# Attention of a fused kernel: scores in blocks of two steps on TensorE, unscaled q prepared on GpSimd

## The chip, the cores and the metric

The kernel runs on one core of one Trainium2 chip. The metric is the device time of one execution in microseconds (us); smaller is better. A core has TensorE (PE in the profile; its weight loads are PEld), VectorE (DVE), ScalarE (ACT), GpSimd (POOL) and SyncE (SP, which here only issues transfers). Each engine runs its own instructions in order, and waits on semaphores for the others.

## The reference

Three stages follow each other: a bucketed attention, a mixture of experts, and a token and channel mixing. Only the attention is touched:

```python
q_bits = (np.einsum('bhsd,dk->bhsk', q, proj) > 0)     # 6 sign bits for each row of q, and of k
mask = q_bucket[:, :, :, None] == k_bucket[:, :, None, :]
scores = scale * np.matmul(q, k.transpose(0, 1, 3, 2)) # scale = 1/8
scores = np.where(mask, scores, -1000000000.0)
scores = scores - np.max(scores, axis=-1, keepdims=True)
attn = np.exp(scores)
attn = attn / (np.sum(attn, axis=-1, keepdims=True) + 1e-09)
return np.matmul(attn, v)
```

There are 2 x 8 = 16 heads, 768 rows each, 64 columns.

## The kernel before

The 16 heads are worked on in 8 pairs. A head has 6 tiles of 128 query rows, so there are 96 steps g. Step g belongs to pair g // 12, to head g % 2 of it and to tile g % 12 // 2; n stands for g % 12. A step goes through four engines:

- PE, `score(g)`: four matmuls write `scores[g % 2]`, 128 query rows by 768 keys. Two multiply `q_aug` by `k_aug` (the high part of 64 columns, and 12 rows of sign bits that push a score far down where the buckets differ), two multiply `q_hl` by `k_lh` (the products of the low parts). It waits for the exponential of step g-2, which read the same buffer.
- DVE, `maximum(g)`: the negated row maximum `neg_max`, then `match` (is there a key in the row's bucket) and `bias`, each one column.
- ACT, `exponential(g)`: exp of `scores` times `match` plus `bias` to `probs[g % 3]`, with the row sums as a by-product.
- PE, `turn(g)`: six transposes of `probs` into `turned`, of which there is one buffer. It waits for the exponential of g and for the copy of g-1 out of `turned`.
- ACT, `evict(g)`: copies `turned` to `probs_t`.
- PE, `products`: 8 matmuls with v into `pv` in every odd step, for steps 8 and 9 back. Every six steps DVE copies `pv` to `out_t` (`evict_out`, at n = 2 and 8), PE turns that into `side` (`turn_out`, at n = 3 and 9), and DVE normalises it into `x_all`.

The order on ACT is written out: in iteration g first `evict(g - 2)`, then `exponential(g)`. The change leaves it as it is. The order on PE is `score(g)`, `turn(g - 2)`, and at odd g the products.

The next pair is prepared while the present one runs. GpSimd starts when the last scores of the pair before are done (`s_sc`), and makes `q_hl` (q times 1/8, rounded), the copies of k (`k_aug`, and half of `k_lh`) and `k_low`, for both heads. DVE makes `q_aug` and `q_low` (the low part of q) between its maxima. PE projects q and k on the bit directions at n = 5 (`Q_AT`) and n = 7 (`K_AT`) into `side`, and DVE turns them into bits (`signs`) at n = 5 and 6 for q, and at n = 7 and 8 for k; each call has two instructions (L268). Before PE writes `side` again, at n = 7 and in `turn_out`, `side_free` waits until the signs counted so far are read out of it:

```python
        def side_free(g):
            turns = (Q_AT < g % 12) + (K_AT < g % 12)
            pe.wait_ge(s_bits, min(8 * (1 + g // 12) + 4 * turns, 8 * NPAIRS))
```

The first pair is prepared apart, most of it on DVE, before the first step.

## Time and profile before

| | before |
|---|---|
| median of 3 runs | 756.32 us (755.98 to 756.4) |
| the profiled execution | 756.28 us, of which span 754.5 us |
| PE busy | 649.6 us (86%) |
| DVE busy | 441.1 us (58%) |
| ACT busy | 350.2 us (46%) |
| POOL busy | 290.3 us (38%) |
| first and last score matmul | 17.7 and 259.3 us |

The attention is the stretch up to about 273 us. Busy shares are of the whole span. A busy PE isn't PE at its peak, since matmuls are pipelined and their ends are modelled; the starts in the timeline are the better guide.

### The profile page before, as it was taken

To read this page: it belongs to the slowest core of one execution; us is meant where nothing else is said; L and a number is where in the kernel's file an instruction comes from. 1 tells how busy PE (TensorE), PEld (TensorE's weight loads), DVE (VectorE), ACT (ScalarE), POOL (GpSimd) and SP (SyncE) were. 2 spreads that over 40 slices of the span, in tenths; PEclk is the share of its full clock that TensorE was granted. 3 is DMA by queue.
4 is the path that set the end of the run, shared out by engine and by line. 5 is a ranking of instruction groups with operands and counts; after the bars stand their busy time and mean duration, and the time that the engine had idled before them with its cause. 6 is when DMAs were issued, how large, how long until landed. Compare 5 with 4: busy or idle time off the path is not lost. (4 is left out here: it accounts for less than half of the span.)

```text
span 754.5 us, 10408 instructions
## 1 busy us (share of the span) xinstructions
PE 649.6 (86%) x3742; PEld 513.0 (68%) x3743; DVE 441.1 (58%) x736; ACT 350.2 (46%) x528; POOL 290.3 (38%) x163
## 2 busy tenths in 40 slices
PE   2899999999999979207999999999477899799998
PEld 0666666666666659107889998899365678678886
DVE  6788888888886421703466545561368885632222
ACT  2677676776767723004245543451245554622100
POOL 3360632605420026252366444660255655733300
PEclk9999999999999995557999999999888999989999
DMA  9103261541615035244676566711442102122311
GB/s 297 53 1 120 97 217 25 193 145 73 217 57 189 1 149 214 83 172 164 223 252 217 201 212 232 250 45 42 142 173 77 56 1 84 42 84 84 111 43 56
DMA packets 50975, 96.09 MB, mean 127 GB/s; under 512 B 16624, under 2 KB 16624, under 8 KB 50928
## 3 DMA queue, kind: packets, MB, share of 16 engines
q1 hardware_dynamic: 48720, 88.38, 34.4%
q0 software_dynamic: 1920, 6.29, 2.4%
q10 hardware_dynamic: 288, 0.79, 0.3%
q8 instruction: 30, 0.49, 0.3%
q14 instruction: 17, 0.14, 0.1%
HBM read 69.23 MB, written 26.21 MB: 127 GB/s over the span
## 5 line engine op out<-in xcount | busy, mean ns | idle before, releaser
L835 POOL TENSOR_TENSOR w_lo<-stage,w_hi 128x1024 fp32r<-128x1024 f32 x28 | 85.2, 3064 | 86.7 <-ACT w_hi L830 86.7
L221 ACT ACTIVATE probs<-scores,bias,match 128x768 f32<-128x768 f32 x96 | 95.5, 994 | 43.6 <-DVE bias L281 43.6
L275 DVE TENSOR_REDUCE neg_max<-scores 128x1 f32<-128x768 f32 x96 | 91.2, 950 | 22.4 <-PE scores L377 19.8
L213 ACT COPY probs_t<-turned 128x768 f32<-128x768 f32 x96 | 76.5, 797 | 39.2 <-PE turned L386 38.0
L386 PE MATMUL turned<-ident,probs 128*128 128x128 f32 x576 | 81.2, 278 | 9.7 <-ACT probs_t L213 9.6
L386 PEld LDWEIGHTS turned<-ident,probs 128*128 128x128 f32 x576 | 66.0, 142 | 24.8 <-issue 23.0
L924 PE MATMUL up<-xt_hi,w_hi 128*128 128x256 f32 x256 | 73.4, 287 | 3.6 <-DVE xt_lo L877 2.0
L168 POOL TENSOR_SCALAR q_hl<-q_raw 128x768 fp32r<-128x768 f32 x14 | 33.5, 2394 | 111.0 <-PE scores L377 110.1
L924 PE MATMUL up<-xt_hi,w_lo 128*128 128x256 f32 x256 | 73.1, 286 | 0.0
L924 PE MATMUL up<-xt_lo,w_hi 128*128 128x256 f32 x256 | 73.1, 286 | 0.0
L398 PE MATMUL pv<-probs_t,v_in 128*64 128x384 f32 x384 | 72.3, 498 | 0.8 <-DVE out_t L288 0.8
L377 PE MATMUL scores<-k_aug,q_aug 76*128 76x384 f32 x192 | 60.1, 395 | 11.6 <-DVE k_aug L268 9.0
L1262 PE MATMUL y<-z_hi,wt_hi 128*128 128x512 f32 x144 | 58.1, 403 | 8.7 <-POOL wt_lo L1046 5.9
L835 DVE TENSOR_TENSOR w_lo<-stage,w_hi 128x1024 fp32r<-128x1024 f32 x28 | 54.3, 1940 | 6.0 <-ACT w_hi L830 5.3
L1262 PE MATMUL y<-z_lo,wt_hi 128*128 128x512 f32 x144 | 57.3, 398 | 0.0
L1262 PE MATMUL y<-z_hi,wt_lo 128*128 128x512 f32 x144 | 57.0, 396 | 0.0
L830 ACT CAST w_hi<-stage 128x1024 fp32r<-128x1024 f32 x56 | 55.7, 1046 | 0.0
L377 PEld LDWEIGHTS scores<-k_aug,q_aug 76*128 76x128 f32 x192 | 30.0, 196 | 36.1 <-issue 18.5
L863 ACT ACTIVATE ht_hi<-up 128x512 fp32r<-128x512 f32 x32 | 19.2, 600 | 73.6 <-PE up L924 73.6
L1052 POOL TENSOR_TENSOR z<-z,x_tok 128x512 f32<-128x512 f32 x24 | 35.4, 1496 | 46.5 <-ACT z L1108 46.5
L924 PEld LDWEIGHTS up<-xt_hi,w_hi 128*128 128x128 f32 x256 | 49.9, 195 | 2.7 <-DVE xt_lo L877 2.4
L1046 POOL TENSOR_TENSOR wt_lo<-wt_raw,wt_hi 128x1536 fp32r<-128x1536 f32 x11 | 39.4, 3584 | 31.6 <-ACT wt_hi L1076 31.6
(161 smaller groups left out, 1377.5 us busy)
## 6 DMA issues: line engine op xcount, KB each, us to landing
stage<-in_w SPq DMA_DIRECT2D x64, 512.0 KB, 4.8
wt_raw<-in_w_tok SPq DMA_DIRECT2D x12, 768.0 KB, 4.4
x_slots<-zeros SPq DMA_DIRECT2D x7, 1024.0 KB, 8.9
y_slots<-zeros SPq DMA_DIRECT2D x7, 1024.0 KB, 11.2
q_raw<-in_qT SPq DMA_DIRECT2D x16, 384.0 KB, 5.3
k_raw<-in_kT SPq DMA_DIRECT2D x14, 384.0 KB, 6.0
x_in<-x_slots SPq DMA_DIRECT2D x10, 512.0 KB, 5.0
y_slots<-y_out SPq DMA_DIRECT2D x8, 512.0 KB, 2.8
```

The costliest lines, as they stand in the source:

```text
L213: nc.scalar.copy(probs_t[j % 2][:, a, :, t % 3 * P:(t % 3 + 1) * P].rearrange("k (b n) q -> k b n q", b=2), turned[:, :, 0:HALF].rearrange ...
L221: nc.scalar.activation(probs[g % 3][:].rearrange("p (b n) -> p b n", b=2), scores[g % 2][:, :, 0:HALF], ACT.Exp, bias=bias[:, pair, a, t:t ...
L275: nc.vector.tensor_reduce(neg_max[:, pair, a, t:t + 1], scores[g % 2][:, :, 0:HALF], AX.XY, ALU.max, negate=True).then_inc(s_neg, 1)
L377: last = nc.tensor.matmul(scores[g % 2][:, half, 0:HALF], qq[:, rows], kk[:, half * HALF:half * HALF + HALF], start=n == 0, stop=n == 1)
L386: last = nc.tensor.transpose(turned[:, k // 3, k % 3 * P:(k % 3 + 1) * P], probs[g % 3][:, k * P:(k + 1) * P], ident[:])
L398: last = nc.tensor.matmul(pv[a * D:(a + 1) * D, 0:HALF], v_in[pair % 2][:, a, k, :], probs_t[j % 2][:, a, k, :], start=k == 0, stop=k == T ...
L830: nc.scalar.copy(w_hi[w][:, r, :], stage[:, r, :]).then_inc(s_wh, 1)
L835: name.tensor_tensor(w_lo[w][:, r, :], stage[:, r, :], w_hi[w][:, r, :].bitcast(F32), ALU.subtract).then_inc(done, 1)
L924: last = nc.tensor.matmul(up[f // 2][:, f % 2, :], (w_hi, w_lo)[b][w][:, k, f * P:(f + 1) * P], (xt_hi, xt_lo)[a][:, k, :], start=k == 0 a ...
L1046: nc.gpsimd.tensor_tensor(wt_lo[i % 3][:], wt_raw[:], wt_hi[i % 3][:].bitcast(F32), ALU.subtract).then_inc(s_wtl, 1)
L1052: nc.gpsimd.tensor_tensor(z[m][c % 2][:], z[m][c % 2][:], x_tok[:, c, :], ALU.mult).then_inc(s_z, 1)
L1262: last = nc.tensor.matmul(y[n % 4][:], (wt_hi, wt_lo)[a][n % 3][:, m, s, :], (z_hi, z_lo)[w][:, c, m, :], start=s == 0 and m == 1 and k == ...
```

## The change

PE works in blocks of two steps. At an even g it turns step g-2 first, and then computes the scores of g and of g+1; at g+1 it turns g-1 and does the products. DVE takes both maxima of a block, those of g and g+1, at the even g, and what belonged between them (the signs of n = 5 to 8) comes behind both. q isn't scaled any more: the factor 1/8 goes into the scale of the exponential (`scale` takes the place of `match`), and `bias` becomes `neg_max` times `scale`, so that it waits for `scale`; the constants for mismatches are 8 times as large. For the next pair GpSimd now makes `q_hl`, `q_aug`, `q_low`, and the three parts of k. In the first pair DVE, ACT and GpSimd share the work, the projection matrix is loaded ahead of q, and the first step waits for the signs of its own head alone.

```diff
     @block.sync
-        load_rows(sp, q_raw, qT, 0, 0)
         sp.dma_start(proj_raw[:], proj).then_inc(s_const_ld, 16)
-        load_rows(sp, q_raw, qT, 0, 1)
+        for a in range(2):
+            load_rows(sp, q_raw, qT, 0, a)
...
     @block.gpsimd
         def q_high(pair, a):
             p = pair % 2
             pool.wait_ge(s_klo, 2 * pair + a)
             pool.wait_ge(s_qk[p][a], 32 * (pair // 2) + 32)
-            nc.gpsimd.tensor_scalar(q_hl[p][a][:], q_raw[p][a][:], SCALE, None, ALU.mult).then_inc(s_qhi, 1)
+            nc.gpsimd.tensor_copy(q_hl[p][a][:], q_raw[p][a][:]).then_inc(s_qhi, 1)
+
+        def q_augment(pair, a):
+            p = pair % 2
+            pool.wait_ge(s_qhi, 2 * pair + a + 1)
+            pool.wait_ge(s_qaug, 2 * pair + a)
+            nc.gpsimd.tensor_copy(q_aug[p][a][0:D, :], q_raw[p][a][0:D, :]).then_inc(s_qaug, 1)
+
+        def q_low(pair, a):
+            p = pair % 2
+            pool.wait_ge(s_qaug, 2 * pair + a + 1)
+            pool.wait_ge(s_qlo, 2 * pair + a)
+            nc.gpsimd.tensor_tensor(q_hl[p][a][D:P, :], q_raw[p][a][D:P, :], q_hl[p][a][D:P, :].bitcast(F32),
+                                    ALU.subtract).then_inc(s_qlo, 1)
...
-        k_low(0, 1)
+        for a in range(2):
+            k_low(0, a)
...
                 for a in range(2):
                     q_high(pair + 1, a)
+                    q_augment(pair + 1, a)
+                    q_low(pair + 1, a)
                     k_high(pair + 1, a)
                     k_low(pair + 1, a)
...
     @block.scalar
+        act.wait_ge(s_kaug, 1)
+        nc.scalar.copy(k_aug[0][1][0:D, :], k_raw[0][1][0:D, :]).then_inc(s_kaug, 1)
+        act.wait_ge(s_qaug, 1)
+        nc.scalar.copy(q_aug[0][1][0:D, :], q_raw[0][1][0:D, :]).then_inc(s_qaug, 1)
...
     @block.vector
         def maximum(g):
...
-            dve.wait_ge(s_neg, g + 1)
-            nc.vector.tensor_scalar(match[:, pair, a, t:t + 1], neg_max[:, pair, a, t:t + 1], -FLOOR, None,
-                                    ALU.is_le).then_inc(s_max, 1)
-            nc.vector.scalar_tensor_tensor(bias[:, pair, a, t:t + 1], neg_max[:, pair, a, t:t + 1], -FLOOR,
-                                           neg_max[:, pair, a, t:t + 1], ALU.is_le, ALU.mult).then_inc(s_max, 1)
+            dve.wait_ge(s_neg, 2 * g + 1)
+            nc.vector.tensor_scalar(scale[:, pair, a, t:t + 1], neg_max[:, pair, a, t:t + 1], -FLOOR, SCALE,
+                                    ALU.is_le, ALU.mult).then_inc(s_neg, 1)
+            dve.wait_ge(s_neg, 2 * g + 2)
+            nc.vector.tensor_tensor(bias[:, pair, a, t:t + 1], neg_max[:, pair, a, t:t + 1],
+                                    scale[:, pair, a, t:t + 1], ALU.mult).then_inc(s_max, 1)
...
             if g < STEPS:
-                maximum(g)
+                if g % 2 == 0:
+                    maximum(g)
+                    maximum(g + 1)
                 if pair + 1 < NPAIRS:
-                    if n in (3, 10):
-                        q_low(pair + 1, n // 6)
-                    if n in (1, 4):
...
-                        q_augment(pair + 1, n // 4)
...
     @block.tensor
             if g % 12 < 2:
-                pe.wait_ge(s_bits, 8 * pair + 8)
+                pe.wait_ge(s_bits, 8 * pair + (8 if pair > 0 else 4 * a + 4))
...
-            if g < STEPS:
-                score(g)
-            if 0 <= g - T_LAG < STEPS:
-                turn(g - T_LAG)
-            if 0 <= g - PV_LAG < STEPS and g % 2 == 1:
+            if g % 2 == 0:
+                if 0 <= g - T_LAG < STEPS:
+                    turn(g - T_LAG)
+                for m in (g, g + 1):
+                    if m < STEPS:
+                        score(m)
+            else:
+                if 0 <= g - T_LAG < STEPS:
+                    turn(g - T_LAG)
                 for m in (g - PV_LAG - 1, g - PV_LAG):
-                    products(*divmod(m, 6))
+                    if 0 <= m < STEPS:
+                        products(*divmod(m, 6))
```

The order that comes out of it, at the places that matter. First PE before, n = 6 and 7 of the second pair (a score is two rows, `turned` is the transposes, `pv` the products, `side` the projection of k):

```order
L377 MATMUL scores<-k_aug,q_aug 128x384 x2
L377 MATMUL scores<-k_lh,q_hl 128x384 x2
L386 MATMUL turned<-ident,probs 128x128 x6
L377 MATMUL scores<-k_aug,q_aug 128x384 x2
L377 MATMUL scores<-k_lh,q_hl 128x384 x2
L386 MATMUL turned<-ident,probs 128x128 x6
L398 MATMUL pv<-probs_t,v_in 64x384 x4
L350 MATMUL side<-k_raw,w_bits 12x384 x4
```

And the same stretch of PE in the changed kernel:

```order
L400 MATMUL turned<-ident,probs 128x128 x6
L391 MATMUL scores<-k_aug,q_aug 128x384 x2
L391 MATMUL scores<-k_lh,q_hl 128x384 x2
L391 MATMUL scores<-k_aug,q_aug 128x384 x2
L391 MATMUL scores<-k_lh,q_hl 128x384 x2
L400 MATMUL turned<-ident,probs 128x128 x6
L412 MATMUL pv<-probs_t,v_in 64x384 x4
L364 MATMUL side<-k_raw,w_bits 12x384 x4
```

The transposes now stand ahead of the block's first scores, and one score follows the other.

On DVE before, from n = 6 to the maximum of n = 8 (L268 is `signs`, two instructions a call):

```order
L275 TENSOR_REDUCE neg_max<-scores 128x1
L279 TENSOR_SCALAR match<-neg_max 128x1
L281 SCALAR_TENSOR_TENSOR bias<-neg_max 128x1
L268 TENSOR_SCALAR q_aug<-side,thresh_q 12x384 x2
L275 TENSOR_REDUCE neg_max<-scores 128x1
L279 TENSOR_SCALAR match<-neg_max 128x1
L281 SCALAR_TENSOR_TENSOR bias<-neg_max 128x1
L268 TENSOR_SCALAR k_aug<-side,thresh_k 12x384 x2
L288 COPY out_t<-pv 128x384
L275 TENSOR_REDUCE neg_max<-scores 128x1
```

The same stretch of DVE in the changed kernel:

```order
L294 TENSOR_REDUCE neg_max<-scores 128x1
L298 TENSOR_SCALAR scale<-neg_max 128x1
L301 TENSOR_TENSOR bias<-neg_max,scale 128x1
L294 TENSOR_REDUCE neg_max<-scores 128x1
L298 TENSOR_SCALAR scale<-neg_max 128x1
L301 TENSOR_TENSOR bias<-neg_max,scale 128x1
L287 TENSOR_SCALAR q_aug<-side,thresh_q 12x384 x2
L287 TENSOR_SCALAR k_aug<-side,thresh_k 12x384 x2
L308 COPY out_t<-pv 128x384
L294 TENSOR_REDUCE neg_max<-scores 128x1
```

The second call of q's signs has moved behind the second maximum of its block, and k's first call follows it at once.

## Rows read from the trace of the kernel before

**Rows 1.** Busy time by engine in stretches: one pair (31 us), all after the attention.

```profile
106.33:137.37 31.04, 29.74 (x192) 19.46 (x192) 26.57 (x55) 21.78 (x37) 11.73 (x8) 1.00 0.40 131
...
274.00:754.50 480.50, 405.84 (x2222) 353.11 (x2222) 228.24 (x280) 171.68 (x234) 205.05 (x99) 0.90 0.39 134
```

**Rows 2.** Timeline of one block: start, duration, engine, line, operation, idle before.

```profile
139.43 0.62 PE L377 MATMUL scores<-k_aug,q_aug 76*128 76x384 f32 x2
...
139.88 0.52 PE L377 MATMUL scores<-k_lh,q_hl 128*128 128x384 f32 x2
...
140.24 0.82 PE L386 MATMUL turned<-ident,probs 128*128 128x128 f32 x6
140.44 0.96 DVE L275 TENSOR_REDUCE neg_max<-scores 128x1 f32<-128x768 f32 x1 [1.39 <-PE scores L377]
...
140.81 0.60 PE L377 MATMUL scores<-k_aug,q_aug 76*128 76x384 f32 x2
...
141.09 0.80 ACT L213 COPY probs_t<-turned 128x768 f32<-128x768 f32 x1 [0.92 <-PE turned L386]
...
141.43 0.15 DVE L279 TENSOR_SCALAR match<-neg_max 128x1 f32<-128x1 f32 x1
141.50 0.15 DVE L281 SCALAR_TENSOR_TENSOR bias<-neg_max 128x1 f32<-128x1 f32 x1
141.79 1.00 ACT L221 ACTIVATE probs<-scores,bias,match 128x768 f32<-128x768 f32 x1
...
142.04 0.84 PE L386 MATMUL turned<-ident,probs 128*128 128x128 f32 x6 [0.27 <-ACT probs_t L213]
142.68 0.20 ACT L221 ACTIVATION_READ_ACCUMULATOR probs<-scores,bias,match 128x1 f32 x1
...
142.82 1.51 PE L398 MATMUL pv<-probs_t,v_in 128*64 128x384 f32 x8
...
144.26 0.62 PE L377 MATMUL scores<-k_aug,q_aug 76*128 76x384 f32 x2
```

**Rows 3.** Timeline around the signs of k, n = 7 to 10.

```profile
128.73 0.83 PE L350 MATMUL side<-k_raw,w_bits 64*12 64x384 f32 x8
...
129.63 1.25 DVE L268 TENSOR_SCALAR k_aug<-side,thresh_k 12x384 fp32r<-12x384 f32 x2 [0.54 <-PE side L350]
...
130.92 0.56 DVE L288 COPY out_t<-pv 128x384 f32<-128x384 f32 x1
...
132.62 1.27 DVE L268 TENSOR_SCALAR k_aug<-side,thresh_k 12x384 fp32r<-12x384 f32 x2
...
134.33 0.55 PE L406 MATMUL side<-ident,out_t 128*128 128x128 f32 x3
```

**Rows 4.** Timeline, GpSimd's instructions and three of DVE's bias.

```profile
137.37 2.43 POOL L168 TENSOR_SCALAR q_hl<-q_raw 128x768 fp32r<-128x768 f32 x1 [18.53 <-PE scores L377]
...
138.91 0.15 DVE L281 SCALAR_TENSOR_TENSOR bias<-neg_max 128x1 f32<-128x1 f32 x1
...
141.79 1.81 POOL L183 TENSOR_TENSOR k_lh<-k_raw,k_aug 64x768 fp32r<-64x768 f32 x1 [0.15 <-POOL k_lh L176]
...
142.87 0.75 DVE L281 SCALAR_TENSOR_TENSOR bias<-neg_max 128x1 f32<-128x1 f32 x1
...
146.21 0.82 POOL L174 CAST k_aug<-k_raw 64x768 fp32r<-64x768 f32 x1
...
146.33 0.71 DVE L281 SCALAR_TENSOR_TENSOR bias<-neg_max 128x1 f32<-128x1 f32 x1
```

**Rows 5.** Timeline of the start: first scores, first exponential, first transposes.

```profile
12.56 2.45 DVE L260 SCALAR_TENSOR_TENSOR q_hl<-q_raw,q_hl 64x768 fp32r<-64x768 f32 x1
...
17.68 1.01 PE L377 MATMUL scores<-k_aug,q_aug 76*128 76x384 f32 x2 [8.97 <-DVE k_aug L268]
...
20.87 0.99 ACT L221 ACTIVATE probs<-scores,bias,match 128x768 f32<-128x768 f32 x1 [11.96 <-DVE bias L281]
...
23.45 1.48 PE L386 MATMUL turned<-ident,probs 128*128 128x128 f32 x6
```

More of the change, by code:

```diff
@@ L22 @@
 KAUG = BITS + 2 * NBITS
-MISMATCH = 2.0 ** 35
-FLOOR = -(2.0 ** 33)
+MISMATCH = 2.0 ** 38
+FLOOR = -(2.0 ** 36)
 SCALE = 1.0 / 8.0
@@ L65, in attention @@
     total = sb("total", [P, NPAIRS, 2, T])
-    match = sb("match", [P, NPAIRS, 2, T])
+    scale = sb("scale", [P, NPAIRS, 2, T])
     bias = sb("bias", [P, NPAIRS, 2, T])
@@ L172, in k_high @@
             pool.wait_ge(s_qk[p][a], 32 * (pair // 2) + 32)
-            pool.wait_ge(s_qhi, 2 * pair + a + 1)
+            pool.wait_ge(s_qlo, 2 * pair + a + 1)
             nc.gpsimd.tensor_copy(k_aug[p][a][0:D, :], k_raw[p][a][0:D, :]).then_inc(s_kaug, 1)
@@ L182, in k_low @@
                 pool.wait_ge(s_khi, 2 * pair + a + 1)
+            elif a == 1:
+                pool.wait_ge(s_klo, 1)
             nc.gpsimd.tensor_tensor(k_lh[p][a][0:D, :], k_raw[p][a][0:D, :], k_aug[p][a][0:D, :].bitcast(F32),
                                     ALU.subtract).then_inc(s_klo, 1)
-        k_low(0, 1)
+        for a in range(2):
+            k_low(0, a)
         pool.wait_ge(s_qhi, 2)
@@ L203, in _ @@
             act.wait_ge(s_qk[0][a], 32)
-            nc.scalar.activation(q_hl[0][a][:], q_raw[0][a][:], ACT.Copy, scale=SCALE).then_inc(s_qhi, 1)
+            nc.scalar.copy(q_hl[0][a][:], q_raw[0][a][:]).then_inc(s_qhi, 1)
             nc.scalar.copy(k_lh[0][a][D:P, :], k_raw[0][a][D:P, :]).then_inc(s_khi, 1)
+        act.wait_ge(s_kaug, 1)
+        nc.scalar.copy(k_aug[0][1][0:D, :], k_raw[0][1][0:D, :]).then_inc(s_kaug, 1)
+        act.wait_ge(s_qaug, 1)
+        nc.scalar.copy(q_aug[0][1][0:D, :], q_raw[0][1][0:D, :]).then_inc(s_qaug, 1)
         def evict(g):
@@ L217, in exponential @@
             pair, a, t = place(g)
-            act.wait_ge(s_max, 2 * g + 2)
+            act.wait_ge(s_max, g + 1)
             if g >= 3:
@@ L221, in exponential @@
             nc.scalar.activation(probs[g % 3][:].rearrange("p (b n) -> p b n", b=2), scores[g % 2][:, :, 0:HALF], ACT.Exp,
-                                 bias=bias[:, pair, a, t:t + 1], scale=match[:, pair, a, t:t + 1],
+                                 bias=bias[:, pair, a, t:t + 1], scale=scale[:, pair, a, t:t + 1],
                                  accum_out=total[:, pair, a, t:t + 1]).then_inc(s_exp, 1)
@@ L250, in _, with q_augment, q_low @@
         assert n_const[0] == N_CONSTS
-        def q_augment(pair, a):
-            p = pair % 2
-            dve.wait_ge(s_qk[p][a], 32 * (pair // 2) + 32)
-            nc.vector.tensor_scalar(q_aug[p][a][0:D, :], q_raw[p][a][0:D, :], SCALE, None, ALU.mult).then_inc(s_qaug, 1)
-        def q_low(pair, a):
-            p = pair % 2
-            dve.wait_ge(s_qhi, 2 * pair + a + 1)
-            nc.vector.scalar_tensor_tensor(q_hl[p][a][D:P, :], q_raw[p][a][D:P, :], SCALE, q_hl[p][a][D:P, :].bitcast(F32),
-                                           ALU.mult, ALU.subtract).then_inc(s_qlo, 1)
+        def q_augment(a):
+            nc.vector.tensor_copy(q_aug[0][a][0:D, :], q_raw[0][a][0:D, :]).then_inc(s_qaug, 1)
+        def q_low(a):
+            dve.wait_ge(s_qhi, a + 1)
+            nc.vector.tensor_tensor(q_hl[0][a][D:P, :], q_raw[0][a][D:P, :], q_hl[0][a][D:P, :].bitcast(F32),
+                                    ALU.subtract).then_inc(s_qlo, 1)
         def signs(pair, a, of_k, src):
@@ L305, in normalise @@
                                     ALU.mult).then_inc(s_norm, 1)
+        dve.wait_ge(s_qk[0][0], 32)
+        nc.vector.tensor_copy(k_aug[0][0][0:D, :], k_raw[0][0][0:D, :]).then_inc(s_kaug, 1)
+        q_augment(0)
         for a in range(2):
-            dve.wait_ge(s_qk[0][a], 32)
-            nc.vector.tensor_copy(k_aug[0][a][0:D, :], k_raw[0][a][0:D, :]).then_inc(s_kaug, 1)
-            q_augment(0, a)
-            q_low(0, a)
-            if a == 0:
-                dve.wait_ge(s_kaug, 1)
-                nc.vector.tensor_tensor(k_lh[0][0][0:D, :], k_raw[0][0][0:D, :], k_aug[0][0][0:D, :].bitcast(F32),
-                                        ALU.subtract).then_inc(s_klo, 1)
+            q_low(a)
             for of_k in range(2):
@@ L324, in _ @@
             if g < STEPS:
-                maximum(g)
+                if g % 2 == 0:
+                    maximum(g)
+                    maximum(g + 1)
                 if pair + 1 < NPAIRS:
-                    if n in (3, 10):
-                        q_low(pair + 1, n // 6)
-                    if n in (1, 4):
-                        if n == 1 and pair > 0:
-                            dve.wait_ge(s_sc, 12 * pair)
-                        q_augment(pair + 1, n // 4)
                     if n in (Q_AT, K_AT):
@@ L335, in _ @@
                     if n in (Q_AT, Q_AT + 1, K_AT, K_AT + 1):
+                        if n == Q_AT and pair > 0:
+                            dve.wait_ge(s_sc, 12 * pair)
                         signs(pair + 1, (n - Q_AT) % 2, n // K_AT, side)
```

## Prediction

> **What bounds the kernel now.** I read the busy time in stretches first. A pair takes 31.04 us, and PE is busy for 29.74 of them, DVE for 26.57, ACT for 21.78, GpSimd for 11.73 [rows 1]. What comes behind the attention, 480.5 us, isn't touched and only moves. So the question is how long a pair gets.
>
> Then the timeline of one block of two steps [rows 2]. The block begins with the scores at 139.43 and the next begins at 144.26: 4.83 us. By starts, PE spends 0.81 on the first score, 0.57 on the transposes, about 0.80 on the second score, then it stands for 0.27 (and its pipeline runs empty, together some 0.4) until ACT has copied `turned`, then 0.78 on the second transposes and 1.44 on the products. Six blocks are 29.0; the projections of q and k (0.8 each) and two `turn_out` (0.3 each) make 31.2, the measured pair. So PE's own order bounds a pair, with one stall of 0.4 a block. Everything else has slack: the exponential starts at 141.79, 0.14 after its bias, and no score waits for it.
>
> **The loop that the new order closes.** The change aims at the stall: between the two transposes there are now two scores (1.6 us) instead of one, and the copy (0.80) fits in. PE's own content is 0.57 + 0.81 + 0.80 + 0.78 + 1.44 = 4.40 a block. But the transposes of g now stand ahead of the scores of g+2, and they wait for `evict(g - 1)`; ACT's order, which stays, puts that copy behind `exponential(g)`. Before, `score(g + 2)` stood ahead of that wait. Now, counted from the start of `turn(g - 2)`, with the durations of [rows 2]:
>
> - score g starts at 0.60 (0.57 in the row), and ends 0.97 later (139.43 to 140.40), at 1.57;
> - 0.04 on, DVE's maximum of 0.96 ends at 2.57; 0.03, then `scale` 0.15: 2.75;
> - `bias` now waits for `scale`. Before it began 0.07 behind `match`; now it begins behind its end, some 0.02 later, and ends at 2.92. That is 0.10 more than before;
> - the hand-over to ACT I take as 0.04, like that from PE to DVE; the exponential starts at 2.96. With the accumulator's read it holds ACT for 1.09 (141.79 to 142.88): 4.05;
> - `evict(g - 1)`, 0.80: 4.85; then 0.15 to the transposes (141.89 to 142.04): 5.00.
>
> So a block takes 5.0 us, not 4.83, and PE stands for 0.6 of it. The stall isn't removed but moved to the block's head, and grown. The other waits hold no longer: the exponential of g-1 ends near 0.95, ahead of score g+1 at 1.4; `evict(g - 2)` ends at 1.75, ahead of the second transposes at 2.2.
>
> The rule of the Trainium skill (VectorE: DVE Perf Modes, section on the DRAIN) speaks otherwise on the third step: in a chain of DVE instructions "the semaphore costs nothing extra". The row shows `bias` starting while `match` still runs [rows 2], so the trace doesn't bear it out here. By the page a block would be 4.9.
>
> **Where the signs have gone.** Blocks at n = 0, 2 and 10 take 5.0. In the block n = 4/5 PE has 4.40 + 0.8 for q's projection: 5.2. In n = 6/7 q's second signs come behind both maxima: the second maximum runs from 2.85 to 3.81, its small ones to 4.1, the signs (1.27, as in [rows 3]) to 5.4. PE reaches `side_free` for k's projection at 4.4 and waits for them: 5.5, and with the projection 6.3. In the trace before, this projection starts at 128.73 with no wait [rows 3]. k's first signs start 0.9 after the projection (128.73 to 129.63), so they end 1.4 into the next block; `evict_out` (0.56) follows on DVE, so that the maximum of n = 8 starts at 2.0 instead of 1.6. Late next are that block's bias, exponential and copy, each by 0.4; k's second signs end at 5.8, `turn_out` waits for them (before they ended at 133.89, ahead of it at 134.33 [rows 3]), and the block takes 6.2. The pair: 3 x 5.0 + 5.2 + 6.3 + 6.2 = 32.7 us.
>
> **GpSimd.** DVE loses two `q_augment` and two `q_low` a pair; it has slack in ordinary blocks, so I count this at nothing. What they cost now is something else. The bias, 0.15 long when nothing is in its way, took 0.75 and ended at 143.62, with GpSimd's subtraction ending at 143.60; another took 0.71 and ended at 147.04, with GpSimd's copy ending at 147.03. But one at 138.91 ran its 0.15 in the middle of GpSimd's TENSOR_SCALAR of 2.43 [rows 4]. So copies and two-input subtractions hold back DVE's two-input instruction until they end, and the scaled `q_hl` didn't. The new bias has two inputs too. The change takes that harmless instruction away and puts three that hold in its place: per pair 4 subtractions of 1.81 and 8 copies of 0.82, 13.8 us, against 2 and 4, some 6.9, before. The copy of 128x768 is in no row; its bounds are 0.82 (the 64x768 copy) and 2.43 (the scaling it replaces), and I take 0.82, the same operation. GpSimd needs 15 us with its gaps, and has 31. It starts at the end of the pair's last scores, so it covers the bias that leads a block in three blocks. A bias that falls at random into it waits for what is left of an instruction, on the mean (8 x 0.82 x 0.82 + 4 x 1.81 x 1.81) / (2 x 13.8) = 0.67 us, and in the loop nothing absorbs it: 2.0 us a pair. From below it is 0, if each falls into a gap, from above 3 x 1.8 = 5.4. The pair comes to 34.7, 3.7 more than before; for six pairs 22 us.
>
> **First and last pair.** Before, the first scores start at 17.68 and the first exponential at 20.87 [rows 5]. With head 1's share off their way (its signs, 2.5, its `q_low`, which took 2.45, and its copies) the scores start near 12 and, since DVE still does head 1's signs ahead of the first maximum, the first exponential near 16.5: 4.3 gained. It is given back in the same pair. PE runs its first matmuls at half pace (a turn of 1.48 against 0.82 [rows 5, 2]), the turn now stands in the loop, so the first blocks cost about 1.8 more together; the waits at the signs of n = 6/7, and GpSimd, cost 1.3 and 2. Before, this pair had no products in most blocks (1.44 each), which shortened it; now the loop keeps it at 5.0. I take +1 net (from -4 to +3). The last pair has no signs and no GpSimd work: six blocks of 5.0 against 4.83 and two `turn_out` that now hide: 0.4, gone again in the tail, where one turn fewer waits.
>
> **Sum.** 22 + 1 = 23 us, added to the profiled execution's 756.28 (span 754.5 and 1.8 around it), which stands within 0.1 of the median: 779 us.
>
> **The rivals.**
> - *PE's own content decides.* If the copy of g-1 were out before the exponential of g, a block would be PE's 4.40, a pair 6 x 4.40 + 2.2 = 28.6, and with 7 such pairs and 3 us at the start the time 756 - 17 - 3 = 736. For it: the stall of 0.27 in every block [rows 2]. Against it: it decides only if the chain from score g to the copy takes less than 4.4, and its rows add up to 5.0. Some slack that I don't see would have to be 0.6. If it is 0.2 to 0.4, it lies between, near 750. Chance 0.12 for both.
> - *It evens out.* The loop gives 4.83 as before, GpSimd falls into gaps, and the start's gain pays for the signs: 756. Chance 0.04.
> - *The loop holds, but only one addition comes.* Signs hidden or GpSimd harmless: loop with signs alone 6 x 1.7 + 1 = 11, 767; loop with GpSimd alone 6 x 1.2 + 1 = 8, 764. If bias starts as early as before, as the page has it, the sum is 48 x 0.1 = 5 less, 774. Together 0.25.
> - *The forecast*, 779: 0.51.
> - *GpSimd at its worst, or PE falls to the half pace.* The first gives 3.4 more a pair, 799. With PE at half pace a block's loop grows by the turn's 0.6 and the score's 0.7, 1.3; on a third of the blocks, 20 us, also 799. Against it: in the rows PE stays at its pace through its stalls, and the granted clock of the pair reads 1.00, the upper of its two levels (2.4 GHz) [rows 1]. Chance 0.08.
>
> **How the numbers follow.** The range reaches from the single additions (764, less 2 for the start) to half of the worst case for GpSimd (791): 762 to 791, which leaves out the faster and even cases and part of the last. About 0.2% either way (1.5 us) is what a measurement can tell from no change. Faster 0.12, within it 0.04, slower 0.84.
>
> **What the profile after would show.** PE's `turned` at even g waits for ACT's `probs_t` about 0.6 us in each block; a block takes 5.0; PE at n = 7 and 9 waits for DVE's `q_aug` and `k_aug` for 1 us; the bias is long three to six times a pair, most while GpSimd runs; first scores near 12 us. If the blocks take 4.4 to 4.6 and `turned` waits for nothing, the loop is wrong and with it the sign.

## The result and the profile after

The changed kernel takes 770.27 us (median of 4 runs, 769.45 to 771.38), the kernel before 756.15 (4 runs, 755.96 to 756.4). The ratio is 1.0188, with a 95% interval of 1.0173 to 1.0204: slower, by 14.1 us. The profiled execution took 769.5 us, with a span of 767.7.

The profile after, its first part: each engine's busy time, with its share of the span, and its instructions.

```profile
PE 645.7 (84%) x3742; PEld 518.3 (68%) x3743; DVE 433.0 (56%) x705; ACT 348.9 (45%) x530; POOL 307.9 (40%) x192
```

PE, DVE and ACT are all less busy than before, GpSimd more (307.9 against 290.3): no engine got more to do that the others wait for. The time is in waits.

Busy time in stretches after, the fourth pair by itself and all that follows the attention; these answer [rows 1].

```profile
117.34:150.30 32.96, 28.72 (x194) 19.70 (x192) 25.17 (x51) 21.34 (x36) 13.88 (x13) 1.00 0.38 125
289.50:767.70 478.20, 405.16 (x2222) 352.76 (x2222) 228.21 (x280) 171.68 (x234) 205.08 (x99) 0.90 0.39 135
```

By the starts of PE's even scores this pair lasts 32.96 us, against 31.04. PE's busy time is 1.0 lower in it, so that PE stands for some 3 us more. I read the blocks of two steps in this way in every trace (n = 0, 2, 4, 6, 8, 10). The second to the sixth pair agree to 0.06 us, and the table has one of them. The seventh differs, since GpSimd prepares nothing behind it: 32.73 after, with 4.87 at n = 10.

| | blocks of a pair, us | pair | first pair | last pair, to n = 10 |
|---|---|---|---|---|
| before | 4.83 5.13 5.56 5.59 5.14 4.80 | 31.04 | 28.60 | 24.72 |
| after | 5.02 5.25 5.08 6.33 6.16 5.11 | 32.96 | 39.25 | 24.43 |

The last transposes start at 263.96 before and at 279.45 after, 15.5 later: first scores 5.5 earlier (17.68, now 12.15), first pair 10.65 longer, six pairs 11.2 longer together, last pair and tail 0.8 shorter. From there to the end of the span it is 490.5 us before and 488.3 after, though nothing there was changed; over the kernels of this study that do the same work it is 488.3 to 492.1. So 2 us between two spans may lie there, and the blocks are the sharper measure.

A block of the last pair, where neither signs nor GpSimd are in the way: its timeline, answering [rows 2].

```profile
262.96 0.84 PE L400 MATMUL turned<-ident,probs 128*128 128x128 f32 x6 [0.52 <-ACT probs_t L235]
...
263.57 0.60 PE L391 MATMUL scores<-k_aug,q_aug 76*128 76x384 f32 x2
...
264.36 0.52 PE L391 MATMUL scores<-k_aug,q_aug 76*128 76x384 f32 x2
...
264.56 0.96 DVE L294 TENSOR_REDUCE neg_max<-scores 128x1 f32<-128x768 f32 x1 [2.29 <-PE scores L391]
...
265.07 0.82 PE L400 MATMUL turned<-ident,probs 128*128 128x128 f32 x6
265.55 0.15 DVE L298 TENSOR_SCALAR scale<-neg_max 128x1 f32<-128x1 f32 x1
265.74 0.16 DVE L301 TENSOR_TENSOR bias<-neg_max,scale 128x1 f32<-128x1 f32 x1
...
265.82 1.51 PE L412 MATMUL pv<-probs_t,v_in 128*64 128x384 f32 x8
265.94 0.99 ACT L243 ACTIVATE probs<-scores,bias,scale 128x768 f32<-128x768 f32 x1 [1.28 <-DVE bias L301]
...
266.82 0.19 ACT L243 ACTIVATION_READ_ACCUMULATOR probs<-scores,bias,scale 128x1 f32 x1
266.92 0.79 ACT L235 COPY probs_t<-turned 128x768 f32<-128x768 f32 x1
...
267.85 0.85 PE L400 MATMUL turned<-ident,probs 128*128 128x128 f32 x6 [0.52 <-ACT probs_t L235]
```

Here the loop can be read off: transposes 262.96, score 263.57, its maximum 264.56, `scale` 265.55, `bias` 265.74 (0.19 after `scale`; before, `bias` started 0.07 after `match`), exponential 265.94, the copy of the step before at 266.92, and the next transposes at 267.85, which waited 0.52 for that copy. A block is 4.89. The stall of 0.27 in the middle of a block is gone: the second transposes (265.07) and the products wait for nothing.

The signs after, n = 7 to 9, in the timeline of the fourth pair; these answer [rows 3].

```profile
136.30 1.27 DVE L287 TENSOR_SCALAR q_aug<-side,thresh_q 12x384 fp32r<-12x384 f32 x2
...
137.62 0.83 PE L364 MATMUL side<-k_raw,w_bits 64*12 64x384 f32 x8 [1.19 <-DVE q_aug L287]
...
138.52 1.25 DVE L287 TENSOR_SCALAR k_aug<-side,thresh_k 12x384 fp32r<-12x384 f32 x2 [0.95 <-PE side L364]
...
140.28 0.95 DVE L294 TENSOR_REDUCE neg_max<-scores 128x1 f32<-128x768 f32 x1
...
142.89 1.27 DVE L287 TENSOR_SCALAR k_aug<-side,thresh_k 12x384 fp32r<-12x384 f32 x2
...
144.22 0.55 PE L420 MATMUL side<-ident,out_t 128*128 128x128 f32 x3 [1.44 <-DVE k_aug L287]
```

PE reaches the projection of k at 136.43 and stands for 1.19 until DVE has made q's second signs, which stand behind both maxima. It then stands for 1.44 at `turn_out`, for k's.

GpSimd and the bias after, around the start of the same pair, answering [rows 4].

```profile
114.84 0.82 POOL L174 CAST q_aug<-q_raw 64x768 fp32r<-64x768 f32 x1
...
115.69 0.15 DVE L298 TENSOR_SCALAR scale<-neg_max 128x1 f32<-128x1 f32 x1
...
115.74 1.81 POOL L180 TENSOR_TENSOR q_hl<-q_raw,q_hl 64x768 fp32r<-64x768 f32 x1
...
115.88 1.68 DVE L301 TENSOR_TENSOR bias<-neg_max,scale 128x1 f32<-128x1 f32 x1
...
116.74 0.84 PE L400 MATMUL turned<-ident,probs 128*128 128x128 f32 x6 [0.76 <-ACT probs_t L235]
...
119.51 0.16 DVE L301 TENSOR_TENSOR bias<-neg_max,scale 128x1 f32<-128x1 f32 x1
119.53 1.82 POOL L198 TENSOR_TENSOR k_lh<-k_raw,k_aug 64x768 fp32r<-64x768 f32 x1
```

The bias at 115.88 takes 1.68 instead of 0.16 and ends with GpSimd's subtraction (117.55). The one at 119.51 starts 0.02 ahead of such a subtraction and takes 0.16. Five of a pair's twelve are long, this one the longest.

The start after, answering [rows 5].

```profile
12.15 1.01 PE L391 MATMUL scores<-k_aug,q_aug 76*128 76x384 f32 x2 [3.52 <-POOL k_lh L198]
...
16.91 0.60 DVE L301 TENSOR_TENSOR bias<-neg_max,scale 128x1 f32<-128x1 f32 x1
...
17.54 0.99 ACT L243 ACTIVATE probs<-scores,bias,scale 128x768 f32<-128x768 f32 x1 [6.54 <-DVE bias L301]
...
18.61 1.74 DVE L301 TENSOR_TENSOR bias<-neg_max,scale 128x1 f32<-128x1 f32 x1
...
18.67 1.54 PE L400 MATMUL turned<-ident,probs 128*128 128x128 f32 x6 [1.28 <-ACT probs L243]
...
22.71 1.30 DVE L301 TENSOR_TENSOR bias<-neg_max,scale 128x1 f32<-128x1 f32 x1
...
25.97 1.51 PE L400 MATMUL turned<-ident,probs 128*128 128x128 f32 x6 [1.52 <-ACT probs_t L235]
```

The first scores come 5.5 us earlier, the first exponential 3.3 (20.87, now 17.54). The first four bias instructions are all long, 0.60, 1.74, 1.30, and 0.74 at 25.11: GpSimd has already begun the next pair. The transposes at 25.97 still take 1.51, and those at 29.84 1.09; those at 32.09 and 34.19 take 0.84 and 0.82.

PE in the first pair, n = 7 and 8, and the granted clock (the column ahead of the DMA share) in three stretches.

```profile
37.63 1.47 PE L364 MATMUL side<-k_raw,w_bits 64*12 64x384 f32 x8 [2.62 <-DVE q_aug L287]
...
39.03 1.54 PE L400 MATMUL turned<-ident,probs 128*128 128x128 f32 x6
...
42.92 1.36 PE L400 MATMUL turned<-ident,probs 128*128 128x128 f32 x6
...
45.66 0.87 PE L400 MATMUL turned<-ident,probs 128*128 128x128 f32 x6
```

```profile
34.00:37.60 3.60, 1.01 (x8) 0.74 (x7) 3.37 (x8) 2.54 (x4) 0.00 (x0) 0.95 0.02 5
37.60:44.00 6.40, 6.37 (x28) 5.01 (x28) 3.26 (x6) 1.75 (x4) 0.00 (x0) 0.50 0.00 0
44.00:50.00 6.00, 6.00 (x38) 3.64 (x37) 4.26 (x11) 4.03 (x9) 1.84 (x3) 1.00 0.00 0
```

PE worked for 1.01 of 3.60 us, waited for 2.62 at the projection of k, and then had the lower level of its clock (0.50, 1.2 GHz) until about 44. Transposes took 1.54 and 1.36 there, and 0.87 after it.

### The profile page after: what moved, and what is told of

It reads as the page before. It is cut to its first block and busy times, and to the rows that moved or that the text cites. A ratio compares the mean times of both kernels' runs of the same rounds, so it can differ in the third digit from the quotient of the medians.

```text
span 767.7 us, 10437 instructions
## 1 busy us (share of the span) xinstructions
PE 645.7 (84%) x3742; PEld 518.3 (68%) x3743; DVE 433.0 (56%) x705; ACT 348.9 (45%) x530; POOL 307.9 (40%) x192
## 5 line engine op out<-in xcount | busy, mean ns | idle before, releaser
L243 ACT ACTIVATE probs<-scores,bias,scale 128x768 f32<-128x768 f32 x96 | 95.5, 995 | 76.3 <-DVE bias L301 75.8
L400 PE MATMUL turned<-ident,probs 128*128 128x128 f32 x576 | 83.8, 283 | 13.9 <-ACT probs_t L235 12.5
L400 PEld LDWEIGHTS turned<-ident,probs 128*128 128x128 f32 x576 | 67.8, 145 | 39.7 <-ACT probs L243 24.0
L391 PE MATMUL scores<-k_aug,q_aug 76*128 76x384 f32 x192 | 57.3, 381 | 8.1 <-POOL k_lh L198 3.5
L168 POOL CAST q_hl<-q_raw 128x768 fp32r<-128x768 f32 x14 | 12.1, 867 | 111.1 <-PE scores L391 110.5
L391 PE MATMUL scores<-k_lh,q_hl 128*128 128x384 f32 x192 | 52.3, 355 | 0.0
```

What stands on the lines that cost most here:

```text
L243: nc.scalar.activation(probs[g % 3][:].rearrange("p (b n) -> p b n", b=2), scores[g % 2][:, :, 0:HALF], ACT.Exp, bias=bias[:, pair, a, t:t ...
L391: last = nc.tensor.matmul(scores[g % 2][:, half, 0:HALF], qq[:, rows], kk[:, half * HALF:half * HALF + HALF], start=n == 0, stop=n == 1)
L400: last = nc.tensor.transpose(turned[:, k // 3, k % 3 * P:(k % 3 + 1) * P], probs[g % 3][:, k * P:(k + 1) * P], ident[:])
```

## The experiments

All comparisons are with runs of the kernel before on the same chip in the same batch (its medians: 756.17, 756.1 and 755.52). Blocks and pairs are read in the profiled execution of each. The theory that I started with: PE's new order closes the loop, and through it signs and holds become time, so that the old order takes most of the loss away. The rivals: the loss comes from DVE's order (the signs behind both maxima), or from the bias (two inputs, and chained to `scale`), whatever the order on PE. The blocks and pairs are again those of a middle pair.

| | median, us | ratio (95%) | blocks of a pair | pair | first pair |
|---|---|---|---|---|---|
| e1 old PE order | 766.62 | 1.0143 (1.0126 to 1.016) | 4.83 5.13 5.56 6.14 6.13 4.80 | 32.59 | 35.31 |
| e2 signs between | 760.86 | 1.0062 (1.004 to 1.0085) | 5.42 5.61 5.09 5.08 5.59 4.93 | 31.72 | 35.67 |
| e3 bias of one input | 757.97 | 1.0027 (1.0016 to 1.0037) | 4.80 4.80 5.09 6.06 5.90 4.80 | 31.43 | 33.43 |
| e4 q back on DVE | 769.73 | 1.0196 (1.017 to 1.0222) | 5.42 4.88 5.08 6.33 6.16 5.11 | 32.98 | 35.69 |
| e6 e2 and e3 | 751.03 | 0.9933 (0.9908 to 0.9957) | 4.80 4.80 5.83 5.09 5.25 4.80 | 30.56 | 32.15 |
| e7 e6, old PE order | 752.13 | 0.9942 (0.992 to 0.9964) | 4.83 5.13 5.56 5.59 5.12 4.80 | 31.03 | 30.30 |
| e8 bias unchained | 767.6 | 1.0159 (1.0132 to 1.0185) | 4.80 5.48 5.09 6.08 5.91 5.16 | 32.52 | 36.36 |
| e9 first pair alone | 752.69 | 0.9957 (0.9943 to 0.9972) | 4.83 5.13 5.56 5.59 5.14 4.80 | 31.04 | 31.70 |
| e10 e6, no addition | 745.04 | 0.9872 (0.9846 to 0.9898) | 4.80 4.80 5.08 5.09 5.24 4.80 | 29.82 | 32.15 |

### e1: PE's old order in the changed kernel

```diff
-            if g % 2 == 0:
-                if 0 <= g - T_LAG < STEPS:
-                    turn(g - T_LAG)
-                for m in (g, g + 1):
-                    if m < STEPS:
-                        score(m)
-            else:
-                if 0 <= g - T_LAG < STEPS:
-                    turn(g - T_LAG)
+            if g < STEPS:
+                score(g)
+            if 0 <= g - T_LAG < STEPS:
+                turn(g - T_LAG)
+            if g % 2 == 1:
```

> The changed kernel with TensorE's order of before (score g, turn g-2, score g+1, turn g-1, products); all else as changed. Theory 1 (the loss of an ordinary block comes from the transposes standing ahead of the block's scores and behind ScalarE's copy, and most of the waits for the signs too, since the second score comes later there only by 0.6 us but the block ends later): an ordinary block is TensorE's own 4.8 us again, the waits for the signs shrink from 1.2 to about 0.3 us, a pair takes 31.0 to 31.8 us and the kernel 753 to 758 us. Rival (GpSimd's copies and the chained bias are the loss, whatever TensorE's order): a pair stays above 32.3 us and the kernel above 765 us.

Measured: 766.62, where my theory gave 753 to 758. The theory fell. The old order takes 0.37 us off a pair and 3.9 off the first, no more. The pair is still 1.55 longer than before, and all of it is in the blocks of n = 6 and 8 (6.14 against 5.59, 6.13 against 5.14). The timeline of e1 at the signs:

```profile
132.20 1.27 DVE L287 TENSOR_SCALAR q_aug<-side,thresh_q 12x384 fp32r<-12x384 f32 x2
...
133.52 0.83 PE L364 MATMUL side<-k_raw,w_bits 64*12 64x384 f32 x8 [0.47 <-DVE q_aug L287]
...
140.12 0.55 PE L420 MATMUL side<-ident,out_t 128*128 128x128 f32 x3 [0.94 <-DVE k_aug L287]
```

PE waits at both places in the old order too, for 0.47 and 0.94. This run also shows what a long bias costs in the old order. In the blocks of n = 0 and 2 of the fourth pair:

```profile
116.17 1.47 DVE L301 TENSOR_TENSOR bias<-neg_max,scale 128x1 f32<-128x1 f32 x1
...
119.64 1.67 DVE L301 TENSOR_TENSOR bias<-neg_max,scale 128x1 f32<-128x1 f32 x1
120.06 0.85 PE L400 MATMUL turned<-ident,probs 128*128 128x128 f32 x6 [0.28 <-ACT probs_t L235]
```

The blocks of n = 0, 2 and 10 are those of before (4.83, 5.13, 4.80): there the hold costs nothing. They are 0.6 shorter together than in the changed kernel, but that of n = 4 is 0.48 longer (5.56 against 5.08). The projection of q adds 0.73 to a block in the old order (5.56 against 4.83) and 0.19 in the new one (5.08 against 4.89), where most of it fits into the stall.

### e2: the signs between the maxima

```diff
-                if g % 2 == 0:
-                    maximum(g)
-                    maximum(g + 1)
+                maximum(g)
```

> The changed kernel with one maximum a step on VectorE again, so that each call of the signs stands behind one maximum and not behind two; TensorE's new order stays. Theory 1: the blocks at n = 6 and 8 fall from 6.3 and 6.2 us to 4.9 to 5.2, a pair from 32.96 to 30.3 to 30.8 us, below the 31.04 of before; in the first pair TensorE's wait of 2.6 us goes, and with it the stretch at the lower granted clock; the kernel takes 748 to 753 us. Rival (the maxima of a block stay delayed by the signs now between them, which the loop passes on): a pair at 31.8 to 32.6, the kernel 760 to 768 us.

Measured: 760.86, and a pair of 31.72, 1.24 shorter; both are above what I expected, and the time is in the range of the rival. The blocks of n = 6 and 8 fall from 6.33 and 6.16 to 5.08 and 5.59, by 1.8 together. But those of n = 0 and 2 grow from 5.02 and 5.25 to 5.42 and 5.61. Only DVE's order was changed, so its bias now meets GpSimd's instructions in other places. What the signs gave back, the holds took in part. In the first pair PE's wait at the signs is 1.37 instead of 2.62, its clock doesn't fall, and the pair is 3.6 shorter.

### e3: a bias of one input

```diff
-            dve.wait_ge(s_neg, 2 * g + 2)
-            nc.vector.tensor_tensor(bias[:, pair, a, t:t + 1], neg_max[:, pair, a, t:t + 1],
-                                    scale[:, pair, a, t:t + 1], ALU.mult).then_inc(s_max, 1)
+            nc.vector.tensor_scalar(bias[:, pair, a, t:t + 1], neg_max[:, pair, a, t:t + 1], SCALE, 16.0,
+                                    ALU.mult, ALU.min).then_inc(s_max, 1)
```

The exponential waits for `scale` too. The bias is no longer 0 in a row without a match, but at most 16; there `scale` is 0, all columns get the same factor, and the division by the row sum takes it out.

> The changed kernel with bias worked out from neg_max alone (times 1/8, at most 16), a TENSOR_SCALAR with one input that waits for nothing new; where a row has no key of its bucket, scale is 0 and the bias 16, which cancels in the division. Theory 1 (in the loop nothing absorbs what the bias adds: 0.1 to 0.15 us of chaining a block, and GpSimd's hold, some 0.7 us a pair): no bias is longer than 0.2 us, an ordinary block takes 4.75 to 4.8, a pair 31.4 to 32.0 and the kernel 758 to 764 us. Rival (the one-input instruction is held by GpSimd as well, or another wait takes its place): long ones stay, the kernel at 767 us or more.

Measured: 757.97, with a pair of 31.43, as expected. All 96 bias instructions have one duration, as the group of this tile shows (minimum, median and maximum in ns):

```profile
L301 DVE TENSOR_SCALAR bias<-neg_max x96: 143/144/146, 16.8 to 261.6; 128x1 f32<-128x1 f32 x96
```

The blocks of n = 0, 2 and 10 are 4.80. So what they had above 4.80 came from the bias: chained to `scale`, and held by GpSimd. The blocks of the signs stay at 6.06 and 5.90.

### e8: two inputs, not chained

The same as e3, with a bias that reads a second input (a column of 16.0) for nothing.

```diff
+            nc.vector.scalar_tensor_tensor(bias[:, pair, a, t:t + 1], neg_max[:, pair, a, t:t + 1], SCALE,
+                                           sixteen[:], ALU.mult, ALU.min).then_inc(s_max, 1)
```

> The changed kernel with bias as a two-input instruction that doesn't wait for scale: neg_max times 1/8, at most a column that holds 16. It separates what the kernel with a one-input bias took away together, the chaining and GpSimd's hold. Theory 2 (the hold is the larger part in pairs 0 to 6, the chaining the whole in the last): the last pair's blocks 4.80 as with one input, but the bias still long five times a pair, a pair 32.3 to 32.8 us against 31.43 with one input, and the kernel 765 to 769 us. Rival (the chaining is the larger part): a pair below 31.8 and the kernel below 761 us.

Measured: 767.6, pair 32.52, both as expected. Against e3 only the second input differs: 1.09 a pair is the hold's price, most of it in the blocks of n = 2 and 10 (5.48 and 5.16 against 4.80). Two of the middle pairs begin with 5.02 and 5.23 instead of 4.80 and 5.48, so the holds can fall in more than one way. The instruction that adds 1e-9 to the row sums takes 0.81 instead of 0.16 in six pairs of e8, but in the fourth pair DVE then waits 0.82 for PE's next scores, so that it costs nothing there. Against the changed kernel the chain differs: 0.08 in each block of the last pair (4.81 against 4.89), where no hold is. The 0.44 of a middle pair isn't the chain's alone, since the holds fall elsewhere too. The group of this tile in e8:

```profile
L303 DVE SCALAR_TENSOR_TENSOR bias<-neg_max,sixteen x96: 147/150/1798, 16.8 to 270.7; 128x1 f32<-128x1 f32 x96
```

### e4: q's copies and low parts back on DVE

`q_augment` and `q_low` of the next pair go back to DVE, at n = 1, 4 and n = 3, 10 as before:

```diff
     @block.gpsimd
...
-                    q_augment(pair + 1, a)
-                    q_low(pair + 1, a)
...
     @block.vector
...
+                    if n in (3, 10):
+                        q_low(n // 6, pair + 1)
+                    if n in (1, 4):
...
+                        q_augment(n // 4, pair + 1)
```

> The changed kernel with q_augment and q_low of the next pair back on VectorE, where they stood before (n = 1 and 4, n = 3 and 10), q unscaled; GpSimd has 4 instructions a head instead of 6, some 9 us a pair instead of 14. Theory 2 (the hold by GpSimd costs an unlucky bias, the waits for the signs the rest): the blocks at n = 6 and 8 stay at 6.1 to 6.4, those while GpSimd runs lose 0.2 to 0.7 together, but the copy of q on GpSimd still holds the bias; a pair 32.3 to 33.0, the kernel 764 to 770 us. Rival (the two more instructions a head on GpSimd are most of the loss): a pair below 31.8 and the kernel below 761 us.

Measured: 769.73, the same as the changed kernel, with a pair of 32.98 against 32.96. GpSimd does 9.5 us of work in 33 instead of 13.9, and no bias takes over 0.75 us instead of 1.74, but the block of n = 0 is 5.42 instead of 5.02, that of n = 2 4.88 instead of 5.25. The instructions that the change moved to GpSimd cost the pair nothing that the same work on DVE doesn't cost. The first pair is 3.6 us shorter, yet the median isn't lower, and the stretch behind the attention is 490.1 us in e4's profiled execution against 488.3; I can't say why, beyond that this stretch varies.

### e5: half an exponential

```diff
-            nc.scalar.activation(probs[g % 3][:].rearrange("p (b n) -> p b n", b=2), scores[g % 2][:, :, 0:HALF], ACT.Exp,
+            nc.scalar.activation(probs[g % 3][:].rearrange("p (b n) -> p b n", b=2)[:, :, 0:HALF // 2], scores[g % 2][:, :, 0:HALF // 2], ACT.Exp,
```

It leaves out the exponential of half of the columns, so that what follows the attention works on other data; only the attention is read (the execution as a whole took 834.98 us, once).

> The changed kernel with the exponential of only the first half of each bank's columns (384 of 768 columns of a row); the other columns of probs keep a constant written once at the start, so the attention's output is another one, and the routing behind it too: only the attention's stretch is compared. Theory 1 (an ordinary block is the chain turn, score, maximum, scale, bias, exponential, copy, turn): the exponential gets 0.32 us shorter, and so does the ordinary block, from 4.89 to 4.55 to 4.6 us. Rival (TensorE's own content, or VectorE, sets it): 4.85 us or more, as now.

Measured in the last pair: blocks of 4.56 to 4.65 instead of 4.89. The timeline:

```profile
256.96 0.67 ACT L243 ACTIVATE probs<-scores,bias,scale 128x384 f32<-128x384 f32 x1 [1.28 <-DVE bias L303]
...
257.62 0.79 ACT L235 COPY probs_t<-turned 128x768 f32<-128x768 f32 x1
...
258.55 0.85 PE L402 MATMUL turned<-ident,probs 128*128 128x128 f32 x6 [0.20 <-ACT probs_t L235]
```

The exponential is 0.32 shorter (0.67), the blocks are 0.24 to 0.33 shorter: so the exponential is in the loop. Still `turned` waits 0.20 for ACT. In the blocks with signs nothing changes (6.33, 6.16). Nor does it in those of n = 0 and 2 (5.02, 5.22): there two held bias instructions take longer, 0.76 and 0.81 instead of 0.45 and 0.52, and end with the same GpSimd instructions as in the changed kernel. So while a bias is held, GpSimd's own sequence sets the pace.

### e6, e7 and e10: without the two causes

e6 is e2 and e3 together, e7 is e6 with PE's old order.

> The changed kernel with both: one maximum a step on VectorE (signs between them), and bias from neg_max alone (one input, at most 16). Theory 2 (what the change loses is the waits for the signs, and the bias held by GpSimd and chained to scale; TensorE's new order by itself is no loss once these are gone, since it hides the projections in its slack): ordinary blocks 4.80, those with a projection 5.08, a pair 29.7 to 30.3 us against 31.04 before, no stretch at the lower granted clock after the first 28 us, the kernel 745 to 751 us. Rival (with the signs between them the second maximum is late again, and passes it on through ScalarE): a pair above 30.8, the kernel 753 us or more.

> The same with TensorE's order of before as well. What is left of the change is the first pair, unscaled q, and the preparation on GpSimd. Theory 2: TensorE's own order bounds again, blocks of 4.83, 5.13, 5.56, 5.59, 5.14, 4.80, a pair 31.05 us; only the start is gained: 751 to 754 us, slower than the kernel with the new order by 6 x 1. Rival (the new order is a loss as forecast): this one is the faster of the two, or equal.

Measured: 751.03 and 752.13, both faster than before. e7's time and pair came as expected. e6's pair is 30.56, above the 29.7 to 30.3 expected, and e7 is only 1.1 slower than e6, where 6 was expected. In e7 every block has its length of before, to 0.02 us. In e6 the blocks of n = 0, 2 and 6 are shorter than in e7, but that of n = 4 is 5.83. Its timeline:

```profile
112.44 1.82 POOL L180 TENSOR_TENSOR q_hl<-q_raw,q_hl 64x768 fp32r<-64x768 f32 x1
...
112.65 0.14 DVE L301 TENSOR_SCALAR bias<-neg_max 128x1 f32<-128x1 f32 x1
112.71 1.58 DVE L314 TENSOR_SCALAR recip<-total 128x12 f32<-128x12 f32 x1
...
114.47 0.90 DVE L295 TENSOR_REDUCE neg_max<-scores 128x1 f32<-128x768 f32 x1
```

The addition of 1e-9 to the 12 row sums, 0.16 long in e3, takes 1.58 and ends with the subtraction, and the maximum behind it comes late. It does so in six pairs, for 1.57 to 1.62. e10 leaves this addition out:

```diff
-            nc.vector.tensor_scalar_add(recip[:], total[:, pair, :, :], 1e-9).then_inc(s_rec, 1)
-            dve.wait_ge(s_rec, 2 * pair + 1)
-            nc.vector.reciprocal(recip[:], recip[:]).then_inc(s_rec, 1)
+            nc.vector.reciprocal(recip[:], total[:, pair, :, :]).then_inc(s_rec, 1)
```

> The kernel with one maximum a step and the one-input bias (751.0 us), without the instruction that adds 1e-9 to the row sums (they are at least about 1, so that the sum in float32 stays the same). In that kernel's trace the 128x12 addition on VectorE took 1.58 us instead of 0.16 and ended with GpSimd's subtraction, and the block at n = 2/3 took 5.8 us instead of 5.08. Theory: it was held by GpSimd; the block at n = 2/3 (5.8) falls to 5.1 or below, a pair from 30.56 to 29.8 to 30.0, the kernel to 745 to 748 us. Rival (the reciprocal, or another instruction, is held in its place): 750 us or more.

Measured: 745.04, ratio 0.9872 (0.9846 to 0.9898), 1.3% faster than before. The block of n = 4 is 5.08, the pair 29.82. The rival, that the reciprocal is held in its place, is out: it lies in the same subtraction, and takes 0.22.

```profile
110.47 1.81 POOL L180 TENSOR_TENSOR q_hl<-q_raw,q_hl 64x768 fp32r<-64x768 f32 x1
...
110.74 0.22 DVE L314 RECIPROCAL recip<-total 128x12 f32<-128x12 f32 x1
```

### e9: the new first pair in the kernel before

The kernel before, with the projection matrix loaded first, head 1's copies on ACT, both `k_low` on GpSimd, and the first step waiting for its own head's signs.

```diff
+        act.wait_ge(s_kaug, 1)
+        nc.scalar.copy(k_aug[0][1][0:D, :], k_raw[0][1][0:D, :]).then_inc(s_kaug, 1)
...
+                pe.wait_ge(s_bits, 8 * pair + (8 if pair > 0 else 4 * a + 4))
```

> The kernel before with the first pair's preparation alone as changed (q still scaled): projection matrix ahead of q, k_low of both heads on GpSimd, the copies of head 1 on ScalarE, the first step waiting for its own head's signs. Theory: first scores near 12.2 instead of 17.7 us, the first exponential at 17 to 17.6 instead of 20.87, and nothing of it given back, since the body is that of before: pairs of 31.04, the kernel 752 to 753.5 us. Rival (GpSimd's work for the second pair now lies in the first steps and holds the bias, and the start is given back): 755 us or more.

Measured: 752.69, 3.4 us faster than before; 2.5 of it are in the trace of the attention, where the second pair's scores start at 43.79 instead of 46.28. The first scores come 5.6 earlier (12.09), and 3.1 of it is given back within the first pair (31.70 against 28.60), which I hadn't expected. This part of the change is a gain, and the order of the rest used it up.

## Why the prediction was right, and where it was off

The direction was right, and PE waits at the places that the prediction named: in the loop and at the signs. But the loop that heads it isn't a loss by itself. PE's old order takes only 0.37 of the 1.92 a pair away (e1), and without the late signs and the two-input bias the new order gains (e6 against e7). What costs is the place of the signs, and the chained and held bias in the loop. The time came out at 770.3, inside the range, 8.7 below the forecast.

- **The loop that the new order closes: right.** PE's `turned` at an even g waits for ACT's copy, 0.52 in the row above, where 0.6 was forecast. e5 shows that the exponential is part of it. **Its size was off**: 4.89, not 5.00. The term that was mis-sized is ACT's 1.09 for the exponential with its accumulator. The copy starts 0.98 after the exponential (265.94, 266.92), while the accumulator is still being read (266.82, 0.19). That is 0.11 a block. And the loop by itself is no loss: the last pair, all loop, is 0.3 shorter than before (24.43 against 24.72), since the two `turn_out` hide in it.
- **`bias` waits for `scale`: right, 0.10 forecast.** The trace has 0.19 between their starts where it had 0.07. e8 measures 0.08 a block in the last pair. In the Trainium skill (VectorE: DVE Perf Modes, the section on the DRAIN) the semaphore costs nothing extra in a chain of eight copies; for these single columns the traces show 0.08 to 0.12.
- **The signs: right in place and size.** 6.3 and 6.2 forecast, 6.33 and 6.16 measured, and PE stands at the two places named, for 1.2 and 1.4. e1 shows that this doesn't hang on PE's order.
- **GpSimd: the step that failed.** "The change takes that harmless instruction away and puts three that hold in its place", 2.0 us a pair for them. In the trace the three blocks without signs or projection (n = 0, 2, 10) have 0.71 above 3 x 4.89; e8 against e3 gives 1.09. And e4, without the moved instructions, takes as long. What costs is that a two-input bias stands in the loop while GpSimd works at all. Before, it had two inputs as well and was long as well (0.75 in [rows 4], 1.60 at most), but no score waited for its exponential; e1 has such instructions of 1.47 and 1.67 in the old order, and its blocks of n = 0 and 2 are those of before. I priced meetings by chance. But the second to the sixth pair run alike, to 0.02 us a block, so they aren't random: one bias slips in 0.02 ahead of a subtraction, another waits 1.5 for one, and a change of order elsewhere (e2) moves them.
- **The first pair: under-sized, +1 forecast, +5.1 measured.** The start gained 5.5, the pair then lost 10.65. Against e3, the same pair is 5.8 longer: 2.8 in its first three blocks and 2.75 in those of n = 6 and 8 (7.53 and 6.07 against 6.06 and 4.80), in which PE has 1.2 GHz after and 2.4 GHz in e3. In the first two of the three, the bias instructions take 0.60, 1.74, 1.30 and 0.74. The third, 0.76 longer (5.56 against 4.79), has no long bias of its own: there PE is slow for longer, with transposes of 1.51 and 1.09 at 25.97 and 29.84, where e3's at 24.53 and 26.62 take 0.85 and 0.82. The fall of the clock was among the rivals, for a third of all blocks; it came at one place. And one term was named but stands in no sum: the loop keeps the six blocks near 5.0 where they took 28.6 together, 1.4 more.
- **The sum.** From 779: six pairs of 197.5 together instead of 6 x 34.7 = 208.2, -10.7 (GpSimd -1.3, the three ordinary blocks -0.33 and n = 4 -0.12 a pair, and 0.2 once, in the seventh); first pair +4.1; last pair and tail -0.8; the stretch behind -2.2. That is 769.4, against 769.5 for the profiled execution. So an over-sized and an under-sized term partly cancel; that the forecast came within 9 us is in part luck. The -2.2 belongs to no term of it.
- **The rivals.** That PE's own content decides, 736, didn't come: the chain is longer than 4.40, as its rows said. Nearest came "only one addition", 764 to 774, in its form of loop and signs with a weak GpSimd. The upper end of the range was meant as half of the worst case for GpSimd; 779 and half of the 20 us is 789, not 791.

The terms aren't independent, which my sum took for granted. e2 alone gives 1.24 a pair and e3 alone 1.53, together 2.40 (e6), and the freed pair met another hold, worth 0.74 (e10). For the same reason PE's new order costs 0.37 a pair in the changed kernel (e1) and gains 0.47 without the two causes (30.56 in e6, 31.03 in e7). What the block order needs here, then, is one maximum at a time on DVE, with the signs between, and a bias of one input that waits for nothing on its own engine.

Left open: why the clock fell in the first pair of the changed kernel, of e1, e4, e5 and e8, where PE waited at the signs for 2.62, 1.92, 2.63, 2.62 and 2.37 us, and not in e3, where it waited for 2.36 (in e2 and e6, 1.37 and 1.24, it didn't fall either); and why e4's earlier attention doesn't show in its median.

## What to carry to other kernels

Before an order is changed so that a stall goes, follow the new order once round, from an engine back to itself, and list what stands in that loop: there, each tiny instruction and each hold of another engine is paid in full, where before it was slack. Don't put side work that another engine waits for behind two results; here one result, then the side work, was better, once the bias had one input (e3 against e6). And when a chain of small per-row instructions decides, give them one input and no wait on their own engine, then read the next hold in the trace, since it moves.
